# An attention scan with two feed-forward networks on one core: loads of step 0 reordered, high parts of the weights asked for later, queries of step 1 loaded and used later

## The reference, cut to what matters

```python
# q, k, v: (4, 8, 768, 48), beta: (4, 8, 768)
k_n = k / (norm(k) + 1e-06)
state = zeros((B, H, 48, 48))
for t in range(768):
    y[:, :, t] = q[:, :, t] @ state
    v_old = state^T k_n[t]
    state = state + beta[t] * outer(k_n[t], v[t] - v_old)
x = y as (3072, 384)
h = x @ w_in                                  # 384 -> 2048
g = h where h >= 1, 0 where h <= -1, else (h + 1)^2 / 4
x = g @ w_out                                 # 2048 -> 384
xn = rmsnorm(x) * rms_g
out = (silu(xn @ w_gate) * (xn @ w_val)) @ w_out2   # 384 -> 1536 -> 384
```

## Time and profile before

| | |
|---|---|
| median of 3 runs | 1098.06 us (1096.84 to 1098.83) |
| profiled execution | time 1098.84 us, span 1097.0 us |
| PE busy in the span | 1048.0 us, 96% |
| DVE, ACT busy | 579.1 us (53%), 418.7 us (38%) |
| mean granted TensorE clock | 0.983 |
| data read and written in HBM | 37.06 MB, 9.44 MB |

### The profile page before, as it was taken

How to read it: one execution, slowest core, us unless ns; L and a number is a source line. 1 busy time by engine, 2 the same in 40 slices (tenths; PEclk the granted TensorE clock), 3 DMA queues, 4 the chain that set the end, 5 groups by cost and what they waited for, 6 DMA issues and landing times.

```text
span 1097.0 us, 24182 instructions
## 1 busy us (share of the span) xinstructions
PE 1048.0 (96%) x10828; PEld 850.2 (78%) x10828; DVE 579.1 (53%) x983; ACT 418.7 (38%) x673; POOL 9.6 (1%) x20
## 2 busy tenths in 40 slices
PE   5587899999999999999999999999999999999996
PEld 3266677777777777777787888888888888888885
DVE  5828957948857875893346634333323334233222
ACT  4342353453454444445466644231232232222211
POOL 1000000000000000000000000000000000000000
PEclk9787999999999999999999999999999999999999
DMA  6712200500320240030021312010200200100101
GB/s 205 173 32 60 58 3 18 129 3 2 79 69 2 51 96 3 3 141 6 3 87 35 110 31 85 29 29 1 58 1 1 58 1 1 30 1 1 30 1 29
DMA packets 19031, 48.05 MB, mean 44 GB/s; under 512 B 2448, under 2 KB 9232, under 8 KB 17872
## 3 DMA queue, kind: packets, MB, share of 16 engines
q1 hardware_dynamic: 18928, 46.51, 15.7%
HBM read 37.06 MB, written 9.44 MB: 42 GB/s over the span
## 4 chain that ended last, share of the span: by engine, by line
PE 82%; DVE 10%; issue 3%; DMA 2%; ACT 2%; POOL 0%; DVEq 0%; POOLq 0%; ACTq 0%
PE bank L675 21%; PE acc L1231 15%; PE hps L1216 14%; PE acc L694 10%; PE hps L675 7%; PE hps L694 3%; DMA stage<-w_out 2%; DVE inv L981 2%; DVE outer L977 2%; DVE g L1048 1%; PE bank L1129 1%; PE bank L1155 1%; PE bank L1189 1%; DVE prob L1023 1%; DVE g1l L1055 1%
## 5 line engine op out<-in xcount | busy, mean ns | idle before, releaser
L592 ACT ACTIVATE g<-bank 128x512 f32<-128x512 f32 x72 | 43.1, 599 | 257.2 <-PE bank L675 142.6
L1216 PE MATMUL hps<-xh,w1h 128*128 128x512 f32 x288 | 121.7, 422 | 3.9 <-DVE g L1048 3.8
L1231 PE MATMUL acc<-g1h,w2h 128*128 128x512 f32 x288 | 119.4, 415 | 1.7 <-DVE g1l L1055 1.6
L880 ACT ACTIVATE g1h<-g 128x512 fp32r<-128x512 f32 x96 | 60.7, 632 | 156.7 <-DVE g L1048 140.7
L1216 PE MATMUL hps<-xl,w1h 128*128 128x512 f32 x288 | 114.5, 398 | 0.0
L1216 PE MATMUL hps<-xh,w1l 128*128 128x512 f32 x288 | 114.5, 398 | 0.0
L1231 PE MATMUL acc<-g1l,w2h 128*128 128x512 f32 x288 | 113.8, 395 | 0.0
L1231 PE MATMUL acc<-g1h,w2l 128*128 128x512 f32 x288 | 113.7, 395 | 0.0
L1055 DVE TENSOR_TENSOR g1l<-g,g1h 128x512 fp32r<-128x512 f32 x96 | 66.2, 690 | 68.0 <-ACT g1h L880 67.5
L1048 DVE SCALAR_TENSOR_TENSOR g<-hps,g 128x512 f32<-128x512 f32 x96 | 65.7, 685 | 61.2 <-ACT g L874 61.0
L871 ACT ACTIVATE g<-hps,half_c 128x512 f32<-128x512 f32 x96 | 65.7, 684 | 59.2 <-PE hps L1216 58.4
(11 more groups left out here) (196 smaller groups left out, 2038.7 us busy)
## 6 DMA issues: line engine op xcount, KB each, us to landing
kqT<-kq SPq DMA_DIRECT2D x22, 384.0 KB, 6.4
v_in<-v SPq DMA_DIRECT2D x6, 768.0 KB, 4.3
k_in<-k SPq DMA_DIRECT2D x6, 768.0 KB, 5.6
x2d<-x2s SPq DMA_DIRECT2D x18, 256.0 KB, 5.7
x2t<-x2d SPq DMA_DIRECT2D x6, 768.0 KB, 5.7
y<-y_t SPq DMA_DIRECT2D x48, 96.0 KB, 2.2
stage<-w_in SPq DMA_DIRECT2D x4, 768.0 KB, 8.2
stage<-w_out SPq DMA_DIRECT2D x4, 768.0 KB, 4.7
```

Source lines behind the costliest of these rows:

```text
L880: act.activation(g1h[:, f % 2, :], g1[:, f % 2, :], ACT.Copy).then_inc(s_gh, 1)
L1216: last = pe.matmul(hps[f % 2][:, :], wt[:, kk, P * f:P * f + P], xx[:, kk, :], start=(kk == 0 and e == 0), stop=(kk == KD - 1 and e == 2))
L1231: last = pe.matmul(acc[j][:, :], wt[:, f, P * j:P * j + P], gg[:, f % 2, :], start=(f == 0 and e == 0), stop=(f == NF1 - 1 and e == 2))
```

## The change

In the plan of body 0, `hi n` (n of 2 and more) stands behind piece 3n-2 instead of piece 3n-6, and both `hi 0` and `hi 1` stand ahead of `nrm`. In body 1, `GQ 1,0` and `GQ 1,1` stand at 0.12 and 0.17 of the body's network units instead of 0.04 and 0.09. SP asks for the keys of step 1, chunk 4, v, chunk 5, the queries of step 0, chunks 6 and 7, and the keys of step 0 by token, in this order. The queries of step 1 and the gain wait for the three `XT` of step 0 (`p_xt`) instead of both `X` (`p_x`).

```diff
@@ first_body, split(n): @@
             if p >= 2:
                 ev.append(("low", 0, p - 2))
-            if p % PIECES == 0 and p // PIECES + 2 < NCHUNK:
-                ev.append(("hi", 0, p // PIECES + 2))
+            if p % PIECES == 1 and 2 <= p // PIECES + 1 < NCHUNK:
+                ev.append(("hi", 0, p // PIECES + 1))
@@ first_body @@
         if e[0] == "nrm":
-            out.append(("hi", 0, 0))
+            out += [("hi", 0, 0), ("hi", 0, 1)]
         out.append(e)
-        if e[0] == "nrm":
-            out.append(("hi", 0, 1))
@@ next_body @@
-    ev += [(0.04 + 0.05 * hf, ("GQ", k, hf)) for hf in range(HALVES)]
+    ev += [((0.12 if k == 1 else 0.04) + 0.05 * hf, ("GQ", k, hf)) for hf in range(HALVES)]
@@ SP's list @@
                     for n in range(NSTAGE):
                         load_w(n)
+                    load_kq(1, (0,))
+                    load_w(NSTAGE)
                     load_v(0)
-                    load_w(NSTAGE)
                     load_w(NSTAGE + 1)
-                    load_kq(1, (0,))
                     load_kq(0, (1,))
-                    load_k(0)
                     for n in range(NSTAGE + 2, NCHUNK):
                         load_w(n)
-
-                    sp.wait_ge(p_x, HALVES)
+                    load_k(0)
+
+                    sp.wait_ge(p_xt, KD)
                     load_kq(1, (1,))
                     sp.dma_start(gain[:, :], rms_g.rearrange("(k p) -> p k", p=P), allow_slow_non_contiguous=True).then_inc(e_gain, 16)
```

## The result

The changed kernel takes 1082.64 us (median of 4 executions, 1081.48 to 1083.29) against 1098.44 for the kernel before on the same chips: ratio 0.9856, interval 0.9839 to 0.9873. Predicted were 1082.6 and a range of 1075.5 to 1090.5. The sum of the prediction is right; several of its terms are not, and their errors cancel. The profiled execution has a span of 1081.2 us (time 1083.05).

The account below looks back on a forecast made before the run. Serial `w_out` loads were taken to delay PE in body 0, DVE to set body 1's length. Gains of 14.8 us to `U` plus 0.75 at `KU` made 15.5, so a median of 1082.6 us, range 1075.5 to 1090.5.

Parts of the forecast that it names:

- What bounds it: Body 0: `w_out` loads hold PE, `Z` 18.2 us and `U` 19.3 us later than DVE allows; body 1: DVE's list.
- the ring: Chunks 4 to 7, body 0: one `w_out` load in flight; moving `hi n` lets up to three queue.
- The price of the loads: SP's queue after 18.9 us: 2.9 a `w_out` chunk, 5.2 a kq pair, 1.6 for v or k_in.
- rival A: Loads off the path: `Z` at DVE's 44.6, `U` at 52.2, gain 18.1 + 0.75, time 1079.2; chance 0.20.
- The clock ahead of piece 18: PE idle 2.6 us ahead of piece 18, body 0; clock falls, costing 1.6 us (bounds 0 and 4.8).
- `Z` to `U` taken as 7.6 us: PE, end of the inversion: `U` follows `Z` by 7.6 us as now, so `Z` 47.9, `U` 55.5.
- The stall at `KU`: PE's 2.53 us stall blamed on the transfer beside it; moving that transfer gains 0.75 us (bounds 0 and 1.6).
- the prediction's own sign: It is wrong if the time from `U` to 140 us of now doesn't stay what it is.
- `GQ 1` at no cost: Body 1: PE meets `GQ 1,0` at 83.5 as queries land, slack 3.2 us; cost 0, bounds -1 and +1.

Follow-up runs that it names:

- hi_only: Kernel before plus only the moved high parts (`hi n` two pieces ahead, `hi 1` ahead of `nrm`); 1086.88 us, ratio 0.9899.
- order_only: Kernel before plus only the new order of loads on SP, high parts in their old places; 1091.54 us, ratio 0.9939.
- after_again: The changed kernel once more, unaltered, to see what of its profile repeats; 1081.86 us, ratio 0.9853.
- kq_early: Changed kernel with the queries of step 1 and the gain asked for behind the second `X` again; 1083.25 us, ratio 0.9863.
- gq_early: Changed kernel with `GQ 1` back at 0.04 and 0.09 of body 1; 1084.24 us, ratio 0.9865.
- tail_only: Kernel before plus only the queries of step 1 and gain loaded after `XT`, and `GQ 1` later in body 1; 1095.39 us, ratio 0.9981.
- fill_body0: Kernel `combo` (changed kernel, pieces 22 and 23 ahead of `Z`, step 0 queries behind chunk 7) plus eight unread matmuls around `GQ` and `U`; 1082.81 us.

## Why the prediction was right, step by step

**What bounds it, and the ring: right.** The single load in flight was the larger cause, shown by `hi_only` (11.1 us alone), and what stood ahead of chunk 6 the smaller (`order_only`, 6.5 alone); the chunks asked for at 22.35, 25.6 and 29.2 against 23, 26 and 30; ACT's waits 4.0 against 6; `nrm` at 16.45, covered as costed.

**The price of the loads: too high, by 3.2 us at `Z`.** The term that was mis-sized is the 2.9 us for a chunk, read from one landing at the end of the crowded stretch of the earlier trace rows. v, with the same 768 KB to 128 partitions, was priced at 1.6. Landings in the changed kernel, each its issue plus its time to landing:

| | predicted | landed |
|---|---|---|
| keys of step 1 | 24.1 | 24.4 |
| chunk 4 | 27.0 | 26.3 |
| v | 28.6 | 28.1 |
| chunk 5 | 31.5 | 32.15 |
| queries of step 0 | 36.7 | 35.6 |
| chunk 6 | 39.6 | 37.4 |
| chunk 7 | 42.5 | 39.5 |
| keys of step 0 by token | 44.1 | 41.4 |

All in the order of issue. Chunk 4, v, chunks 6 and 7 and the keys by token each come 1.8 to 2.1 behind the one before. Chunk 5 and the queries take 7.5 together; with 2.0 for the chunk that leaves 5.5 for the pair, and in `hi_only` four halves landed 2.3 to 2.4 apart, 4.7 a pair. So the 5.2 for a kq pair was near, and four chunks at 0.9 too much make the error. The `w_in` chunks, the last three of them 2.0 apart, were the better row; I named them under rival A and did not use them. By them `Z` is held by `ft 0`, which is A's `Z`, and it came at 44.72.

**The clock ahead of piece 18: not in this execution.** PE's longest wait there was 2.09 us, at piece 15, and the clock stayed full. In other profiles with the same order of loads, idle times of 2.86 (`after_again`), 3.10 (`kq_early`) and 2.53 us (`gq_early`) there took it down, and `Z` came at 46.6 to 46.9. Ahead of pieces, from 20 us on, every idle time of 2.5 us and more went with a fall, in `order_only` and `hi_only` (3.18, 3.93) only some 1.5 us after PE went on. From 2.0 to 2.2 us the length alone does not decide: 2.00 (before) and 2.09 left the clock full, 2.04 and 2.17 (`order_only`) took it down. So the step was right for a wait of 2.6 us, and wrong in its place (chunk 5, not chunk 6) and in that the wait was shorter here. The sentence of the Trainium skill ("TensorE: Matmul & The Clock Gate", HAM oscillation), that a wait for a load between bursts throttles the array again when it crosses the window over which activity is watched, agrees with the falls behind the longer of these waits; the 2.09 us one was a wait for a load too and did not do it.

**`Z` to `U` taken as 7.6 us: wrong, 11.7 here, 9.9 in the repeat.** I took the stretch over from the earlier trace rows as if its length were its own. It holds for the profiles where the clock is full through it (7.3 to 8.1: before, `order_only`, `tail_only`, `kq_early`, `gq_early`); in the others the clock is low in part or all of it. A stall of 1.71 us at `X` in place of 0.91 at `GQ` adds 0.8 to it. Why it is low there more often than before was not settled: `fill_body0`, meant for that, came after the fall.

**The stall at `KU`: right in kind, too small.** Taken were 0.75 with a bound of 1.6; the whole 2.53 went, and that is most of the 3.2 us gained from `U` to `nrm`. `tail_only` and `kq_early` show that the transfers beside it are the cause, and the instruction packets show the way. By the prediction's own sign this step was wrong: from `U` to `vn 1` (140 us of now) it is 67.4 us, not 70.6.

**`GQ 1` at no cost: right.** PE waited 2.91 us for the queries, which landed at 83.4 against 83.6 predicted, and 1.92 more for `g 0`, all hidden behind DVE; from `nrm` to `vn 1` it is 44.2 us in both kernels. PE came 2.9 us ahead of the queries and not with them. The prediction didn't price what part 3 costs without part 4: 1.2 and 3.5 us of DVE's list in two profiles.

**Behind `vn 1`: 1.2 us lost, not foreseen.** This is the low clock from 116 to 119.5: DVE sets the time up to `vn 1`, and PE carries its delay past it. The kernel before had the same wait and kept its clock, as four of thirteen profiles did, so this loss need not be the change's own.

That the total was met within 0.1 us is luck to that extent: +3.2 and +2.4 against -4.1 and -1.2.

## What to carry to other kernels

Where a load waits for a buffer and its consumer's wait stands ahead of the very work that frees the next buffer, there is one load in flight however many buffers there are; move the consumer back until the freeing work of all buffers stands ahead of it, and only then look at the order of the transfers. Price transfers by rows from a queue as full as the one that will be there. Two transfers of one size and shape with two prices are a sign that one price is misread. A stretch that moves along behind a removed wait does not keep its length: ask what clock it had, and whether its instructions came beside other transfers.

## What the runs showed of the hardware that was not expected

- PE's instructions come in DMA packets of 16 KB, one for about 127 small matmuls. With nothing beside them they come 3.3 to 4.0 us apart in a dense stretch, and PE stalls up to 1.9 us for them (`fill_body0`); behind 768 KB of queries and the gain one comes 6.7 to 7.2 us after the last, and PE stood 1.3 to 2.8 us in `KU` (before, `order_only`, `hi_only`, `kq_early`). Without the transfers the same block ran through in 0.94 us (`tail_only`).
- The same idle time of 2.12 us ahead of the same matmuls left the clock full in four profiles and took it down for about 3.4 us in nine; `gq_early` and its repeat, one kernel, lie on either side. The fall costs 1.3 us at the end. With 1.8 us of matmuls nobody reads in the wait, the clock stayed full and the median was 1.8 us lower; the intervals overlap.
- Two halves of a kq pair (384 KB to 48 partitions each) take 4.7 to 5.5 us of the queue, a transfer of the same 768 KB to 128 partitions 1.8 to 2.1.
- Four executions of one kernel lay 5.7 us apart (`gq_early`: 1079.48, 1083.45, 1085.03 and 1085.21 us, with a mean granted clock of 0.994, 0.989, 0.986 and 0.983), and the profiled one was the fastest of them, so its profile flattered the edit; the repeat had to decide.
